# The place of a woven attention unit's pieces in the ScalarE and VectorE step lists of a Strassen-like MLP kernel

## The reference

```python
# attention, per chunk of 32 queries: 8 memory keys, 16 keys to the left, 8 to the right
scores = scale * q_c @ k_full.T
a = exp(scores - max(scores)); a = a / (sum(a) + 1e-9)
out[chunk] = a @ v_full
# layer 0
h = x @ w_in0;  g = where(h > 0, h, exp(min(h, 0)) - 1);  x = g @ w_out0
# layer 1
h = x @ w_in1;  g = s * max(h, 0)**2 + b;                 out = g @ w_out1
```

## Time and profile before

| | |
|---|---|
| median of 3 runs | 1161.1 us (1159.33 to 1165.63) |
| profiled execution | 1168.12 us, span 1166.4 us, mean granted TensorE clock 0.985 |
| PE busy | 1103.1 us (95%) |
| DVE busy | 847.5 us (73%) |
| ACT busy | 771.3 us (66%) |
| POOL busy | 387.8 us (33%) |
| woven units, from the first scores to the last P times v | 126 to 473 us |
| HBM | 259 GB/s over the span |

### The profile page before, as it was taken

The page is one execution under the profiler, slowest core; times in us unless marked ns, Lnnn a source line. Parts: engine busy times, 40 slices in busy tenths (PEclk is TensorE's granted clock), DMA queues, the critical chain, the costliest instruction groups (busy, mean ns, idle before and its releaser), DMA issues.

```text
span 1166.4 us, 18156 instructions
## 1 busy us (share of the span) xinstructions
PE 1103.1 (95%) x5787; PEld 880.9 (76%) x5787; DVE 847.5 (73%) x1258; ACT 771.3 (66%) x1806; POOL 387.8 (33%) x427
## 2 busy tenths in 40 slices
PE   8999878999899999989999999999999999999998
PEld 4667656777677777768788787887887887878876
DVE  5695687458967964996986968859848569666385
ACT  4796776578657857756758667757666366675564
POOL 5688779651232332125276103564000000000000
PEclk9898989999999999999999999999999999999999
DMA  9998999999789889868899779898687666776664
GB/s 212 250 270 252 340 324 322 340 281 301 221 261 248 256 242 260 266 204 316 312 350 353 246 247 374 285 358 271 190 264 237 198 188 192 206 228 183 196 185 158
DMA packets 204055, 302.81 MB, mean 260 GB/s; under 512 B 112824, under 2 KB 121016, under 8 KB 203960
## 3 DMA queue, kind: packets, MB, share of 16 engines
q1 hardware_dynamic: 203960, 301.65, 84.4%
HBM read 226.10 MB, written 75.50 MB: 259 GB/s over the span
## 4 chain that ended last, share of the span: by engine, by line
PE 63%; DVE 6%; DMA 3%; ACT 2%; issue 2%; SPq 0%; POOL 0%; ACTq 0%; DVEq 0%; POOLq 0%
PE ps L1005 31%; PE ps L990 28%; DMA w_ring<-w_scratch 2%; DVE g_lo L1464 2%; ACT ps L1085 1%; DVE X L1381 1%; PE ps L954 1%; PE ps L902 1%; DMA elu<-x_scratch 1%; DVE xc_lo L1374 1%; PE ps L927 1%; ACT elu L1171 1%; DVE y L1381 1%; DVE T L1459 1%; DVE att L1333 0%
## 5 line engine op out<-in xcount | busy, mean ns | idle before, releaser
L990 PE MATMUL ps<-xc_hi,w_ring 128*128 128x512 f32 x1344 | 434.0, 396 | 7.0 <-DVE X L1433 3.8
L1005 PE MATMUL ps<-g_hi,w_ring 128*128 128x512 f32 x1344 | 421.2, 395 | 18.2 <-issue 12.6
L1005 PEld LDWEIGHTS ps<-g_hi,w_ring 128*128 128x128 f32 x1344 | 250.5, 189 | 75.9 <-issue 18.3
L990 PEld LDWEIGHTS ps<-xc_hi,w_ring 128*128 128x128 f32 x1344 | 253.8, 189 | 62.9 <-DVE X L1433 4.3
L990 PE MATMUL ps<-xc_lo,w_ring 128*128 128x512 f32 x672 | 263.2, 392 | 0.0
L1005 PE MATMUL ps<-g_lo,w_ring 128*128 128x512 f32 x672 | 263.0, 391 | 0.0
L788 POOL TENSOR_TENSOR w_new<-w_raw,w_new 128x256 fp32r<-128x256 f32 x179 | 165.6, 930 | 230.8 <-ACT w_new L1224 227.9
L1464 DVE TENSOR_TENSOR g_lo<-X,g_hi 128x512 fp32r<-128x512 f32 x240 | 187.7, 787 | 53.5 <-ACT g_hi L1210 53.0
L1210 ACT ACTIVATE g_hi<-X 128x512 fp32r<-128x512 f32 x240 | 148.8, 628 | 64.4 <-PE ps L1005 62.0
L1381 DVE TENSOR_TENSOR X<-s,ps 128x512 f32<-128x512 f32 x144 | 96.1, 681 | 87.5 <-ACT s L1147 63.6
L1005 PEld LDWEIGHTS ps<-g_lo,w_ring 128*128 128x128 f32 x672 | 126.8, 189 | 27.0
(11 more groups left out here) (117 smaller groups left out, 1340.2 us busy)
## 6 DMA issues: line engine op xcount, KB each, us to landing
w_ring<-w_scratch SPq DMA_DIRECT2D x336, 512.0 KB, 4.3
w_scratch<-w_new SPq DMA_DIRECT2D x179, 256.0 KB, 5.3
w_scratch<-att SPq DMA_DIRECT2D x45, 256.0 KB, 4.9
w_raw<-in_moe_w_in SPq DMA_DIRECT2D x16, 512.0 KB, 6.1
w_raw<-in_moe_w_out SPq DMA_DIRECT2D x16, 512.0 KB, 6.1
x_scratch<-y SPq DMA_DIRECT2D x12, 512.0 KB, 6.4
att<-x_scratch SPq DMA_DIRECT2D x12, 512.0 KB, 7.6
out<-elu SPq DMA_DIRECT2D x24, 256.0 KB, 4.3
```

What stands on the lines that cost most here:

```text
L990: last = nc.tensor.matmul(bank_of(st.pi, st.i), w[:, a, cols], x[:, st.pi, kk, :], start=(st.pi in (P1, P5, P4) and kk == 0 and n == 0), s ...
L1005: last = nc.tensor.matmul(bank_of(st.pi, d), w[:, a, cols], x[:, k % RING, :], start=(st.pi in (P1, P5) + (P4,) * (1 - st.gr) and st.i == ...
```

## The change

In each list g of the main loop, ACT takes the exponentials and its half of the copy of the transposed probabilities at the head of the list, and `place_x` in the middle, between `affine` and `cut_g`. `copy_qT` stays at the end. DVE takes the maximum, the normalising and its half of the copy at the head of the list; `copy_kT` stays at the end. No instruction is added or removed, no wait is changed, and PE, POOL and SP keep their order. The 17 units ahead of the main loop are untouched.

```diff
@@ act, for g in range(STEPS + 2) @@
             for g in range(STEPS + 2):
+                for n, at in woven_at(g):
+                    if at == EXP_E:
+                        exps(n, 0)
+                    elif at == EXP_O:
+                        exps(n, 1)
+                    elif at == P_T:
+                        copy_PT(n)
                 for d, x in duos_at(g):
...
                     if d.t >= TPL:
                         affine(d, pi, i)
+                for n, at in woven_at(g):
+                    if at == PV:
+                        place_x(n)
                 for st in splits_at(g):
                     cut_g(st)
...
                     if at == Q_T:
                         copy_qT(n)
-                    elif at == EXP_E:
-                        exps(n, 0)
-                    elif at == EXP_O:
-                        exps(n, 1)
-                    elif at == P_T:
-                        copy_PT(n)
-                    elif at == PV:
-                        place_x(n)
@@ dve, for g in range(STEPS + 2) @@
             for g in range(STEPS + 2):
+                for n, at in woven_at(g):
+                    if at == MAX:
+                        maximum(n)
+                    elif at == NORM:
+                        normalise(n)
+                    elif at == P_T:
+                        copy_PT(n)
                 for d, x in duos_at(g):
...
                     if at == K_T:
                         copy_kT(n)
-                    elif at == MAX:
-                        maximum(n)
-                    elif at == NORM:
-                        normalise(n)
-                    elif at == P_T:
-                        copy_PT(n)
```

## The result

The changed kernel took 1154.9 us (median of 7 runs, 1152.0 to 1157.6) against 1162.5 us of the kernel before (7 runs, the three of the table above and four more): 7.7 us less, ratio 0.9927 with a 95% interval of 0.9901 to 0.9953. In a later comparison it was 0.9929 (0.9906 to 0.9951). I had forecast 14 us less, 1147.1 us, within 1138 to 1161. The direction and the range held; the gain is a little over half of the forecast.

A forecast was written before the change was run, and what follows sets the result against it. PE's work, idle time and lowered clock bound the kernel, with losses between 126 and 473 us. Terms 5.1 + 4.5 + 2.9 + 2.0 + 3.0 - 3.5 = 14.0 us off the 1161.1 us median gave 1147.1 us, range 1138 to 1161.

The forecast's parts named there:

- Copy of the probabilities: PE's waits before the products of P and v: ACT's copy at the list head starts sooner, gaining 5.1 us.
- Maximum, exponentials, normalising: PE's waits for DVE's normalising, 7.0 us: each piece taken a list's body sooner, gaining 4.5 us.
- Placing: PE's waits for ACT's placing, 4.2 us: placed before the cuts, it gains 2.9 us.
- C11: PE's waits for DVE's activation of C11, 3.3 us: exponentials at the head gain 2.0 us.
- the first four run while ACT waits for the product: ACT before C11's activation: first four exponentials fit in a wait and relus keep their time, behind the 2.0 us gain.
- What is late next: Pieces moved ahead of ACT's cuts and DVE's low parts delay those; cost 3.5 us, bounds nothing to 19.5 us.
- My three places for it: Delays expected around 311 us, at C11's exponential at 375.84 (1.3 us later), and in cuts and low parts behind moved pieces.
- Clock: PE's granted clock in the woven part: shorter waits take back 3.0 of 8.4 us lost, bounds 0 and 8.4.
- The idle time moves on: Rival: engine rates set woven waits, so PE only reaches the next missing low part sooner; 4 us gained, 1157 us; chance 0.20.
- The head of the list blocks: Rival: a wait at the head of ACT's or DVE's list delays all behind it; 8 us slower, 1169 us; chance 0.10.
- More goes than I count: Rival: all 21.0 us for moved pieces and most of C11's go, clock at full speed; 29 us, 1132 us; chance 0.11.
- the signs: If right: PE's waits 21.0 to under 10 us, DVE's before normalising well below 18.5, clock from 165 us above 0.87.

The follow-up runs named there:

- place_only: Kernel before with only the placing moved ahead of ACT's cuts, the other pieces left at the end; ratio 1.0005 to the kernel before.
- chain_copies: Changed kernel with the placing put back at the end of ACT's list; maximum, exponentials, normalising and copies stay at the head; ratio 0.9937 to the kernel before.
- light_exp2: Changed kernel with woven exponentials taken for two heads by one instruction (result not the reference's); ratio 0.9911 to the kernel before.
- chain_only: Kernel before with only maximum, normalising and exponentials moved to the head, copies and placing left at the end; ratio 0.9986 to the kernel before.

## Why the prediction was right, and where it was too high

The bound was read rightly: the loss and the gain stand in the woven stretch. It is 10.0 and 10.6 us shorter in the two pairs of traces. Behind it nothing changed: 708.8 and 708.5 us in the first pair, 706.5 and 706.6 us in the second. The means below are over both pairs.

**Copy of the probabilities, 5.1 us.** In front of L927 it is 9.8 - 3.5 = 6.3 us, a bit more.

**Maximum, exponentials, normalising, 4.5 us.** 7.0 - 1.0 = 6.0 us, more too. The reason I gave, that DVE's idle time before the normalising would fall, is not borne out: 18.5 us before, 16.7 and 15.9 us after. DVE waits nearly as long, but sooner, since exponentials and normalising moved together.

**Placing, 2.9 us.** The case that I worked out came as computed, 2.11 us to 0.83 (1.4 expected):

```profile
215.28 0.58 ACT L1135 ACTIVATE ps<-ps 128x512 f32<-128x512 f32 x1
215.80 0.47 ACT L1105 ACTIVATE att<-ps 128x384 f32<-128x384 f32 x1
...
216.32 0.55 PE L884 MATMUL ps<-ident,att 96*128 96x96 f32 x4 [0.83 <-ACT att L1105]
...
244.28 0.55 PE L884 MATMUL ps<-ident,att 96*128 96x96 f32 x4 [1.81 <-ACT att L1105]
```

But the whole wait, 4.2 and 3.4 us before, is 3.7 and 4.2 us after, as a new one of 1.81 us opened one unit on. This is the step that failed, and not by the placing's own price: place_only and chain_copies show that it is worth 2 to 5 us of its wait. I had taken the terms as independent and added them, with the waits of the kernel before as the ceiling of each. They are links of one chain. A unit's pieces follow each other on PE at fixed steps; a link that stands for 3 us gives the later ones time, and when it goes, PE is at the next link sooner than ACT is. So chain and copies handed some 4.5 us on to the placing (4.2 to 8.7 us in chain_copies), which took 5 back.

**C11, 2.0 us.** 3.8 and 3.6 us before, 4.0 and 3.2 us after: nothing. The step that failed is "the first four run while ACT waits for the product". ACT came late out of its cuts and had no such wait; the eight exponentials stood in front of the activation as before, and light_exp2, whose exponentials take 0.9 us less of ACT for each unit, brought PE's wait from 4.0 and 3.2 down to 1.6 us: their work is a good part of the cause. I had taken free time that the earlier trace rows don't show.

**What is late next, -3.5 us.** In front of the down products 4.4 and 3.7 us became 6.9 and 7.9: -3.3 us in the mean. The size was right, the reasons were not. My three places for it did not come out. Around 311 us PE already waited before, 1.81 us at 309.58 and 1.26 us at 312.47; in the changed kernel it is 2.12 us at 300.02. At the exponential for C11 the new gap is 0.16 us, not over one. And the pieces in front of the cuts are not enough by themselves: chain_only has the exponentials, the maximum and the normalising at the head as well, and the wait for low parts is 4.5 us there. It is 8.2 us only in chain_copies, where PE hardly stands in front of L927 any more (1.8 us). That points to a wait handed on here too, to the low parts, though no run shows it apart. The largest new ones show both: 0.97 us before became 1.68 us at 159.26, which chain_only has too (1.70 us), while the 2.11 us at 184.88 are in chain_copies (2.10 us) and not in chain_only.

**Clock, 3.0 us.** Adding up 40 us times what is missing to 1.00 over the stretches from 125 to 445 us: 8.4 and 11.6 us before, 6.8 and 4.8 us after, 4.2 us less in the mean, with a spread of 2 to 3 us from one execution to the next. What I had read was incomplete: I priced the two waits of 3.23 and 3.51 us, but in the same trace the granted clock also fell behind waits of 2.50 us (at 172.86), 2.11 us (at 226.51) and 2.54 us (at 244.01). In the changed kernel it fell behind 1.97, 2.11, 2.65 and 2.12 us. Waits cut to about 2 us were no safeguard. The stretches behind the 2.11 us at 226.51, before, and behind the 2.12 us at 300.02, after, with the granted clock third from the end:

```profile
226.00:230.00 4.00, 3.49 (x12) 2.82 (x13) 0.00 (x0) 1.56 (x5) 3.52 (x5) 0.62 1.03 409
```
```profile
300.00:304.00 4.00, 3.98 (x11) 3.13 (x12) 3.93 (x9) 3.07 (x12) 0.00 (x0) 0.60 0.82 174
```

**The sum.** PE's idle time in the stretch fell by 6.3 + 6.0 - 0.1 + 0.1 - 3.3 - 0.8 = 8.2 us in the mean, the last term for the waits before the scores and for bank sums, which I did not have. My terms without the clock gave 11.0. The stretch fell by 10.3 us, so 2.1 us came from elsewhere, the clock above all; the granted clock alone would say 4.2. At most 0.7 us of that gap is clock that was low while PE sat idle (granted clock and busy time in windows of half a microsecond); the rest of it stays open. Two terms were too small, by 2.7 us together, and two too large, by 4.9 us. That they partly cancel is luck, and without it the time would lie further from the forecast. The last 2 us, from 10.3 us of the stretch to 7.7 to 8.3 us of the medians, are within the intervals. I had carried the difference of one profiled execution over to the median, and no run here shows whether that holds.

**The rivals.** *The idle time moves on* was the better picture for every part alone (0.14 and 0.11% less time, 0.05% more). For the whole it is not far off either: 1154.9 us lies between my forecast (1140 to 1154) and this rival (1155 to 1160), and 7.7 us between my 14 and its 4. I had put it down as a limit by the rates of the engines, while the time went to the next link of a unit. *The head of the list blocks* is real in size, 1.6 us in the case at 229 us, and didn't decide. POOL's wait for the cuts of the weights is unchanged, 136.3 and 134.3 us up to 480 us. *More goes than I count* would have needed the placing and C11. Of the signs, PE's waits for L1094, L1333 and L1105 with those under "issue" came out (21.0 to 7.9 us, under 10 said) and so did the clock from 165 to 205 us (0.87 to 0.92); DVE's wait in front of the normalising did not.

## What to carry to other kernels

Where one item passes several engines and PE asks for each of its pieces at a fixed place, count the waits along the item: a wait that goes can be handed to the next piece unless that is sooner too. So moving one link can show nothing in the time, and a test of each link alone can undervalue moving them all. Compare more than one measure before you say that the parts add up or don't: here the times and the stretch disagree. A piece at the head of an in-order list costs what stands behind it only as far as that has no slack; measure both sides. And before exponentials or any other work is said to run in a wait, look whether the engine does wait there after it comes out of its last block.

## What the runs showed of the hardware that I had not expected

The same wait doesn't always cost TensorE's clock. PE was idle for 2.52 us at 388 us in the first trace of the kernel before, with a granted clock of 1.00 from 365 to 405 us; in the second it was idle for 2.54 us at the same place, with 0.96 in that stretch, and from 125 to 165 us it was 1.00 in one and 0.95 in the other:

```profile
365.00:405.00 40.00, 37.06 (x201) 29.24 (x200) 34.15 (x50) 29.41 (x79) 10.86 (x11) 0.96 0.82 224
```

The changed kernel shows it too: behind the wait of 2.12 us at 300.02 us the granted clock was 0.60 for 4 us, and in its second trace, behind 2.11 us at the same step (304.09 us), it stayed at 1.00 from 285 to 325 us. So 8.4 and 11.6 us of lost clock belong to one and the same kernel, and a gain of the clock's read from one trace of each is uncertain by as much as it is long.

The part ahead of the woven units ended up to 5 us apart between executions (116.0 to 121.1 us) with the same instructions in it; that is half of what the change brings. Without a measure that leaves it out, the pair of profiled spans (13.6 us apart) would have looked like the forecast of 14.0 us come true.
